# A three-stage attention and feed-forward kernel: a first product row in plain fp32, one division moved from GpSimd to VectorE, and three orders changed

## The chip, the cores and the metric

The kernel runs on one core of one Trainium2 chip. The time is the device time of one launch in microseconds (us). The kernel before takes 1252.05 us, the median of three runs (1251.96, 1252.05, 1252.21).

## The reference

Two inputs, x (8 batches, 8 heads, 512 tokens, 64 wide) and 32 states per batch and head, attend to each other in both directions. The 4352 rows of the result (512 + 32 per batch) go through two feed-forward layers. All is fp32.

```python
def _attn_ref(x, state):
    scores = scale * np.matmul(x, state.transpose(0, 1, 3, 2))      # tokens read states
    a = np.exp(scores - scores.max(-1, keepdims=True))
    a /= a.sum(-1, keepdims=True) + 1e-09
    xread = np.matmul(a, state)
    scores2 = scale * np.matmul(state, x.transpose(0, 1, 3, 2))     # states read tokens
    a2 = ...                                                        # the same softmax
    sread = np.matmul(a2, x)
    return np.concatenate([xread, sread], axis=2)

def _moe_ref(x, w1, w2, w3, w_out):       # 512 -> 1024 -> 1024 -> 512
    return (((x @ w1) * (x @ w2)) @ w3) @ w_out

def _moe2_ref(x, w_in, w_out):            # 512 -> 2048 -> 512
    h = x @ w_in
    return (h - np.tanh(h)) @ w_out
```

## The kernel before, in words

Most matrix products are done in three passes of fp32r: each operand is split into a high part (ScalarE copies it to fp32r) and a low part (VectorE subtracts the high part from the whole), and TensorE adds hi·hi, hi·lo and lo·hi. A product that is not split is written in plain fp32.

The program has four stages.

- **The front** (`stage_front`). It folds w3 @ w_out into one matrix `w34` (1024 x 512) in eight rows of 128, and between the rows it does the attention of the states, one batch e after the other. On TensorE batch e is `scores(e)` (L658, plain fp32), three pieces of product row e (`piece`, L699, 6 matmuls each), `sread_turn(e-1)` (L686), `a2_turn(e)` (transposes, L666), the last piece, `sread(e)` (L678). Row 0 and batch 0 stand ahead of this loop in an order of their own, with transposes of an identity in between (`warm`, L641, and `fill`, L646) that compute nothing that is used.
- ScalarE in batch e: `copy_st` (L474, scores out of PSUM), `exp_a2` (L482), `split_sr(e-1)` (L501), `turn_a2` (L490), `split_w3(e+1)` (L451, high part), `empty_prod(e)` (L462), `copy_sr` (L497). From e = 6 also `split_w` (L470).
- VectorE in batch e: `tokens_max` (L573 and L575, the row maximum that the exponential needs), `tokens_invert` (L581, L583), `split_sr(e-1)` (L588), `split_w3(e+1)` (L552, low part), `empty_prod(e)` (L562). In batches 2 to 5 the softmax of the other direction for batch 0 (the class `Rows`) stands in this list: `vector_turn` and `vector_max` at e = 2, `vector_sub` at 3, `vector_sum` (L167) and `vector_invert` (L172, L174) at 4, `vector_back` (L183) at 5. The product with 1/sum between the last two (L179) is GpSimd's.
- `stage_ys` and `stage_moe1` do the states' product and then, for each batch b, the first feed-forward network with w34. Here too `Rows` prepares the batch after the next, its last step at f = 7 of the eight steps f of a batch.
- `stage_moe2` does the second network and stores the result. The last act is the states' rows: eight stores of 64 KB, four from SyncE's queue (half 0) and four from ScalarE's (half 1, after VectorE's last copy, L1327).

What sets the order: each engine runs its own list in the order in which it is written, and waits on semaphores. No scheduler moves anything. Loads are issued by SyncE in the order of `sync`, each after the wait that frees its place: `load_xT(e)` (L375) waits for `scores`, `load_xs(e)` (L381) for `sread`, `load_w3(r)` (L391) for product row r-2 in its buffer of two.

Of the kernel before, what the change touches and what calls it, by code (L numbers as in the profile page):

```python
# [32 lines left out]
P = 128  # L33
# [39 lines left out]
WARM = 36  # L73
# [59 lines left out]
class Rows:  # L133
# [161 lines left out]
def stage_front(nc, sem, room_a, room_b, room_c, room_o, small, w_at, x_rows, x_cols, state_cols, w1, w2, w3_cols, wo, aT, w34_at, w34,  # L295
# [56 lines left out]
    sT_in, xT_in, xs_in = ([sem(f"{x}_in{n}") for n in range(2)] for x in ("sT", "xT", "xs"))  # L352
    w_hi, w_lo = sem("w_hi"), sem("w_lo")
    w3_in, w3_hi, w3_lo = [sem(f"w3_in{n}") for n in range(2)], sem("w3_hi"), sem("w3_lo")
    first_in = [sem(f"first_in{n}") for n in range(2)]
# [77 lines left out]
    def gpsimd(pool):  # L433
# [5 lines left out]
        for e in range(B):  # L439
            rows.gpsimd_scale(pool, e)  # L440

    def scalar(act):
        def split_first(n):
            act.wait_ge(first_in[n], 16)
            act.activation(w3T[0][0][:, FIRST[n], :], w3r[0][:, FIRST[n], :], ACT.Copy).then_inc(w3_hi, 1)

        def split_w3(r):
            act.wait_ge(w3_in[r % 2], 16 * ((r + 1) // 2))

            after(act, prod_done, r - 1)  # L450
# [6 lines left out]
        def empty_prod(r):  # L457
            act.wait_ge(prod_done, r + 1)
# [85 lines left out]
    def vector(dve):  # L544
        def split_first(n):
            dve.wait_ge(w3_hi, n + 1)
            dve.tensor_tensor(w3T[1][0][:, FIRST[n], :], w3r[0][:, FIRST[n], :], plain(w3T[0][0][:, FIRST[n], :]), ALU.subtract
                              ).then_inc(w3_lo, 1)

        def split_w3(r):  # L550
            dve.wait_ge(w3_hi, r + 2)
# [3 lines left out]
        def split_wo(n):  # L555
            dve.wait_ge(wo_hi, n + 1)
# [863 lines left out]
```

## Time and profile before

| | value |
|---|---|
| median of three runs | 1252.05 us |
| time of the profiled execution | 1251.81 us |
| its span, first to last instruction | 1249.6 us |
| TensorE matmul busy | 1239.4 us, 99% of the span |
| TensorE weight load busy | 1007.1 us, 81% |
| VectorE busy | 795.6 us, 64% |
| ScalarE busy | 548.3 us, 44% |
| GpSimd busy | 16.0 us, 1%, 14 instructions |
| DMA, first tenth of the span | 374, 403, 117 and 21 GB/s in four slices of 31 us |

The span is what the profiler saw between the first and the last instruction of the execution; the time has 2.2 us more around it. TensorE is busy in all of the 40 slices of the page. Its busy share says little of its own rate, since matmuls overlap in the record; what matters in the rows below is when each group of its instructions starts.

### The profile page before, as it was taken

How to read it: one execution, taken by the hardware profiler on the slowest of the kernel's cores; microseconds unless marked ns; L12 is line 12 of the kernel's file. 1: busy time of each engine (PE TensorE's matmuls, PEld its weight loads, DVE VectorE, ACT ScalarE, POOL GpSimd, SP SyncE). 2: the span in 40 equal slices, each digit the busy share in tenths (PEclk: the TensorE clock that was granted, in tenths of full speed). 3: DMA queues.
4: the chain of work that ended last, by engine and by line, in shares of the span. 5: the costliest groups of instructions: out<-in, count | busy, mean ns of one | idle time of the engine just before them, and what ended most of it. 6: DMA issues, size and time to landing. Idle time of an engine off the chain costs nothing. (4 is left out here: it accounts for less than half of the span.)

```text
span 1249.6 us, 17133 instructions
## 1 busy us (share of the span) xinstructions
PE 1239.4 (99%) x6652; PEld 1007.1 (81%) x6652; DVE 795.6 (64%) x1282; ACT 548.3 (44%) x1023; POOL 16.0 (1%) x14
## 2 busy tenths in 40 slices
PE   9999999999999999999999999999999999999998
PEld 6779777777777778888888888888888888888887
DVE  4656556555555444878676676676676776776766
ACT  5663333333333334555444444444444444443443
POOL 0000000000000000000000000000000000000000
PEclk9999999999999999999999999999999999999999
DMA  9930100000000111221101001001001001010000
GB/s 374 403 117 21 65 34 1 35 34 1 34 35 1 68 53 66 93 58 35 51 17 37 16 18 51 1 18 50 0 17 50 8 9 50 17 42 0 8 35 17
DMA packets 18109, 63.75 MB, mean 51 GB/s; under 512 B 1920, under 2 KB 3200, under 8 KB 14080
## 3 DMA queue, kind: packets, MB, share of 16 engines
q1 hardware_dynamic: 17712, 62.59, 13.7%
q8 instruction: 40, 0.66, 0.2%
q10 hardware_dynamic: 336, 0.33, 0.1%
q14 instruction: 21, 0.17, 0.0%
HBM read 45.09 MB, written 17.83 MB: 50 GB/s over the span
## 5 line engine op out<-in xcount | busy, mean ns | idle before, releaser
L1213 ACT ACTIVATE hq<-bank 128x512 f32<-128x512 f32 (+1 forms) x144 | 82.8, 575 | 395.8 <-PE bank L1339 395.8
L1284 DVE TENSOR_TENSOR hw<-hw,hq 128x512 f32<-128x512 f32 (+1 forms) x144 | 95.5, 663 | 194.9 <-ACT hw L1224 194.7
L1339 PE MATMUL bank<-ysp_hi,wi_lo 128*128 128x512 f32 (+1 forms) x576 | 217.2, 377 | 0.0
L1339 PE MATMUL bank<-ysp_lo,wi_hi 128*128 128x512 f32 (+1 forms) x576 | 217.2, 377 | 0.0
L1339 PE MATMUL bank<-ysp_hi,wi_hi 128*128 128x512 f32 (+1 forms) x576 | 217.2, 377 | 0.0
L1365 PE MATMUL wide<-wz_hi,gsp_hi 128*128 128x512 f32 x544 | 212.5, 391 | 1.4 <-DVE gsp_lo L1274 1.3
L1365 PE MATMUL wide<-wz_hi,gsp_lo 128*128 128x512 f32 x544 | 211.8, 389 | 0.0
L1365 PE MATMUL wide<-wz_lo,gsp_hi 128*128 128x512 f32 x544 | 211.8, 389 | 0.0
L1339 PEld LDWEIGHTS bank<-ysp_lo,wi_hi 128*128 128x128 f32 x576 | 108.3, 188 | 20.7
L1339 PEld LDWEIGHTS bank<-ysp_hi,wi_hi 128*128 128x128 f32 x576 | 108.2, 188 | 20.5
L1339 PEld LDWEIGHTS bank<-ysp_hi,wi_lo 128*128 128x128 f32 x576 | 108.3, 188 | 19.9
L1365 PEld LDWEIGHTS wide<-wz_hi,gsp_hi 128*128 128x128 f32 x544 | 102.2, 188 | 23.5 <-DVE gsp_lo L1274 2.8
L1365 PEld LDWEIGHTS wide<-wz_hi,gsp_lo 128*128 128x128 f32 x544 | 102.1, 188 | 21.4
L1365 PEld LDWEIGHTS wide<-wz_lo,gsp_hi 128*128 128x128 f32 x544 | 102.2, 188 | 20.5
L1274 DVE TENSOR_TENSOR gsp_lo<-gb,gsp_hi 128x512 fp32r<-128x512 f32 (+1 forms) x144 | 95.5, 663 | 13.4 <-ACT gsp_hi L1206 0.5
L1038 PE MATMUL wide<-psp_hi,w_hi 128*128 128x512 f32 x256 | 101.4, 396 | 0.1
L1301 DVE COPY_PREDICATED gb<-far,wide 128x512 f32<-128x512 uint8 (+1 forms) x144 | 100.8, 700 | 0.2
L1038 PE MATMUL wide<-psp_lo,w_hi 128*128 128x512 f32 x256 | 99.8, 390 | 0.0
L1038 PE MATMUL wide<-psp_hi,w_lo 128*128 128x512 f32 x256 | 99.6, 389 | 0.0
L1303 DVE TENSOR_TENSOR gb<-bank,gb 128x512 f32<-128x512 f32 (+1 forms) x144 | 95.3, 662 | 5.0
L1291 DVE SCALAR_TENSOR_TENSOR gb<-hw,bank 128x512 f32<-128x512 f32 (+1 forms) x144 | 93.7, 651 | 0.1
L1206 ACT ACTIVATE gsp_hi<-gb 128x512 fp32r<-128x512 f32 (+1 forms) x144 | 86.1, 598 | 3.3 <-DVE gb L1303 3.2
(127 smaller groups left out, 1754.7 us busy)
## 6 DMA issues: line engine op xcount, KB each, us to landing
y_dram<-ysb SPq DMA_DIRECT2D x8, 1024.0 KB, 3.9
out<-ysb SPq DMA_DIRECT2D x8, 1024.0 KB, 4.6
yr<-y_dram SPq DMA_DIRECT2D x28, 256.0 KB, 4.1
xs<-in_x_rows SPq DMA_DIRECT2D x6, 1024.0 KB, 8.6
xT<-in_x_cols SPq DMA_DIRECT2D x5, 1024.0 KB, 9.9
w_raw<-in_moe_w SPq DMA_DIRECT2D x8, 512.0 KB, 8.2
wi_raw<-in_moe_w_in SPq DMA_DIRECT2D x4, 1024.0 KB, 6.7
raw<-in_moe_w_out SPq DMA_DIRECT2D x16, 256.0 KB, 2.6
```

Source lines behind the costliest of these rows:

```text
L1038: mm = pe.matmul(py[c], w34[s][:, f, c * P:(c + 1) * P], psp[t][:, f % 2, :], start=f + m == 0, stop=f == NF1 - 1 and m == LAST)
L1206: act.activation(gsp[0][:, slot, 0:w], gb[:, slot % 2, 0:w], ACT.Copy).then_inc(g_hi, 1)
L1213: act.activation(hq[:, f % 2, 0:w], ph[f % 2][:, 0:w], ACT.Square).then_inc(sq_done, 1)
L1274: dve.tensor_tensor(gsp[1][:, slot, 0:w], g, plain(gsp[0][:, slot, 0:w]), ALU.subtract).then_inc(g_lo, 1)
L1284: dve.tensor_tensor(u, u, q, ALU.mult).then_inc(w2_done, 1)
L1291: dve.scalar_tensor_tensor(g, u, 1.0, h, ALU.add, ALU.mult).then_inc(near_done, 1)
L1301: dve.copy_predicated(g, far[:, f % 2, 0:w], pq[f % 2][:, 0:w]).then_inc(sel_done, 1)
L1303: dve.tensor_tensor(g, h, g, ALU.subtract).then_inc(g_done, 1)
L1339: mm = pe.matmul(ph[f % 2][:, 0:w], wi[s][c][:, f * P:(f + 1) * P], ysp[k][u][c][:, 0:w], start=c + m == 0, stop=c == KC - 1 and m == LAST)
L1365: mm = pe.matmul(po[j], gsp[s][:, f % 4, j * P:(j + 1) * P], wz[u][:, f, :], start=f + m == 0, stop=f == NF2 - 1 and m == LAST)
```

## The change

Six edits, all of them in the lists of instructions:

1. Row 0 of the product (`first`, new) is made of whole tiles in plain fp32 (8 matmuls of 128x512) in place of 24 in fp32r from split tiles. The splits of w3's row 0 are gone (`split_first`, two instructions each on ScalarE and VectorE). `warm` has 20 transposes, not 36; `fill` 6 after `scores(0)`, not 12 and 4. w_out is still split, since rows 1 to 7 use its parts, but its low part, which is written over the whole one, now waits for `first`.
2. SyncE loads x of batch 0 (`load_xT(0)`) ahead of the second part of w3's row 0, `load_xs(0)` ahead of w3's row 1, and the states in two parts: batch 1 alone ahead of `load_xT(1)`, the rest behind it.
3. `load_w3(2)` goes ahead of `load_xT(2)`, and `load_w3(5)` ahead of `load_xT(6)`.
4. On VectorE `split_w3(e+1)` and `split_sr(e-1)` go ahead of the `Rows` steps of batches 4 and 5.
5. The product with 1/sum (L179) is done by VectorE in all eight batches, directly ahead of `vector_back`.
6. Of the last four stores on ScalarE's queue one is issued by SyncE.

On TensorE, the start of the program, first before and then after the change:

```order
1 L641 MATMUL wide<-ident 128x128 x36
2 L699 MATMUL bank<-wos_hi,w3T_hi_75 128x512
3 L699 MATMUL bank<-wos_lo,w3T_hi_75 128x512
4 L699 MATMUL bank<-wos_hi,w3T_lo_77 128x512
5 L699 MATMUL bank<-wos_hi,w3T_hi_75 128x512
6 L699 MATMUL bank<-wos_lo,w3T_hi_75 128x512
7 L699 MATMUL bank<-wos_hi,w3T_lo_77 128x512
8 L658 MATMUL wide<-xT,sT 32x512 x8
9 L646 MATMUL wide<-ident 128x128 x12
```

```order
1 L641 MATMUL wide<-ident 128x128 x20
2 L693 MATMUL bank<-wor,w3r_79 128x512 x2
3 L658 MATMUL wide<-xT,sT 32x512 x8
4 L646 MATMUL wide<-ident 128x128 x6
5 L693 MATMUL bank<-wor,w3r_79 128x512 x4
6 L666 MATMUL wide<-ident,a_72 128x128 x8
7 L693 MATMUL bank<-wor,w3r_79 128x512 x2
8 L678 MATMUL wide<-xs,a2T 32x64 x32
9 L658 MATMUL wide<-aT,sT 32x512 x8
```

The eight fp32 matmuls from `w3r` and `wor` are all of row 0; the first piece of it comes before `scores(0)` as before, the last before `sread(0)`.

On SyncE, the loads from the start of the program to the third x (before, then after):

```order
1 L400 DMA w3r_79<-in_w_cols 128x256
2 L397 DMA wor<-in_moe_w_out 128x2x512
3 L400 DMA w3r_79<-in_w_cols 128x768
4 L375 DMA xT<-in_x_cols 128x2048
5 L397 DMA wor<-in_moe_w_out 128x2x512 x3
6 L391 DMA w3r_80<-in_w_cols 128x1024
7 L381 DMA xs<-in_x_rows 128x2048
8 L411 DMA sT<-in_state_cols 128x896
9 L375 DMA aT<-in_x_cols 128x2x1024
10 L381 DMA aT<-in_x_rows 128x2x1024
11 L375 DMA xT<-in_x_cols 128x2048 [waits scored]
12 L391 DMA w3r_79<-in_w_cols 128x1024 [waits prod_done]
```

```order
1 L403 DMA w3r_79<-in_w_cols 128x256
2 L400 DMA wor<-in_moe_w_out 128x2x512
3 L375 DMA xT<-in_x_cols 128x2048
4 L403 DMA w3r_79<-in_w_cols 128x768
5 L400 DMA wor<-in_moe_w_out 128x2x512 x3
6 L381 DMA xs<-in_x_rows 128x2048
7 L394 DMA w3r_80<-in_w_cols 128x1024
8 L414 DMA sT<-in_state_cols 128x128
9 L375 DMA aT<-in_x_cols 128x2x1024
10 L416 DMA sT<-in_state_cols 128x768
11 L381 DMA aT<-in_x_rows 128x2x1024
12 L394 DMA w3r_79<-in_w_cols 128x1024 [waits first_done]
```

Row 9 of both is x of batch 1 (into a part of `aT`). The states of batches 2 to 7 (128x768) now stand behind it.

On VectorE, batches 4 and 5 of the front, from the end of `tokens_invert(4)` to `tokens_max(6)` (before, then after):

```order
40 L167 TENSOR_REDUCE rsum<-a_94 128x32
41 L172 TENSOR_SCALAR rsum<-rsum 128x32
42 L174 RECIPROCAL rinv<-rsum 128x32
43 L588 TENSOR_TENSOR srs_lo<-wide,srs_hi 128x4x32
44 L552 TENSOR_TENSOR w3T_lo_78<-w3r_80,w3T_hi_76 128x1024
45 L562 TENSOR_TENSOR w_lo<-bank,w_hi 128x512
46 L573 TENSOR_REDUCE tmax<-aT 128x2
...
50 L183 STREAM_TRANSPOSE aT<-a_94 128x2x512
51 L588 TENSOR_TENSOR srs_lo<-wide,srs_hi 128x4x32
52 L552 TENSOR_TENSOR w3T_lo_77<-w3r_79,w3T_hi_75 128x1024
53 L562 TENSOR_TENSOR w_lo<-bank,w_hi 128x512
54 L573 TENSOR_REDUCE tmax<-aT 128x2
```

```order
39 L589 TENSOR_TENSOR srs_lo<-wide,srs_hi 128x4x32
40 L551 TENSOR_TENSOR w3T_lo_78<-w3r_80,w3T_hi_76 128x1024
41 L167 TENSOR_REDUCE rsum<-a_94 128x32
42 L172 TENSOR_SCALAR rsum<-rsum 128x32
43 L174 RECIPROCAL rinv<-rsum 128x32
44 L563 TENSOR_TENSOR w_lo<-bank,w_hi 128x512
45 L574 TENSOR_REDUCE tmax<-aT 128x2
...
50 L551 TENSOR_TENSOR w3T_lo_77<-w3r_79,w3T_hi_75 128x1024
51 L179 TENSOR_TENSOR a_94<-a_94,rinv 128x1024
52 L183 STREAM_TRANSPOSE aT<-a_94 128x2x512
53 L563 TENSOR_TENSOR w_lo<-bank,w_hi 128x512
54 L574 TENSOR_REDUCE tmax<-aT 128x2
```

The steps of `Rows` (a_94, rsum, rinv) stood ahead of w3's low part and stand now between it and the next `tmax`; L179 is new on this engine.

The diff, cut to its core:

```diff
-WARM = 36
+WARM = 20
-    def gpsimd_scale(self, pool, e):
+    def vector_scale(self, dve, e):
...
     def load_w3(eng, r):
-        after(eng, prod_done, r - 1)
+        if r == 2:
+            eng.wait_ge(first_done, 4)
+        else:
+            after(eng, prod_done, r - 2)
...
-        split_first(0)
         split_wo(0)
-        split_first(1)
+        copy_st(0)
         split_wo(1)
-        copy_st(0)
+        exp_a2(0)
         split_wo(2)
+        turn_a2(0)
         split_wo(3)
-        exp_a2(0)
-        turn_a2(0)
         split_w3(1)
...
         def split_wo(n):
             dve.wait_ge(wo_hi, n + 1)
+            dve.wait_ge(first_done, n + 1)
...
-        split_first(0)
         split_wo(0)
-        split_first(1)
+        tokens_max(0)
         split_wo(1)
-        tokens_max(0)
+        tokens_invert(0)
         split_wo(2)
-        split_wo(3)
-        tokens_invert(0)
         split_w3(1)
         empty_prod(0)
+        split_wo(3)
...
+            split_sr(e - 1)
+            if e < NF1 - 1:
+                split_w3(e + 1)
             if e == 4:
                 rows.vector_sum(dve, 0)
                 rows.vector_invert(dve, 0)
             if e == 5:
+                rows.vector_scale(dve, 0)
                 rows.vector_back(dve, 0)
-            split_sr(e - 1)
-            if e < NF1 - 1:
-                split_w3(e + 1)
             empty_prod(e)
...
+        def first(n):
+            pe.wait_ge(first_in[min(n, 1)], 16)
+            pe.wait_ge(wo_in[n], 16)
+            for k in (2 * n, 2 * n + 1):
+                mm = pe.matmul(pz[0], w3r[0][:, k, :], wor[:, k, :], start=k == 0, stop=k == NF1 - 1)
+            mm.then_inc(first_done, 1)
...
                     if f == 7:
+                        rows.vector_scale(dve, b + 2)
                         rows.vector_back(dve, b + 2)
...
         sp.wait_ge(o_copied, J * B + 1)
         store_states(sp, 0)
+        sp.wait_ge(second_copied, 1)
+        store_states(sp, 1, range(3, P // NS))
...
             act.wait_ge(second_copied, 1)
-            store_states(act, 1)
+            store_states(act, 1, range(3))
```

## Rows read from the trace of the kernel before

**Rows 1.** Busy time by stretch: front, first network (engines, PEclk, DMA share, GB/s)

```profile
20.00:30.00 10.00, 9.63 (x129) 6.70 (x129) 4.09 (x8) 6.30 (x14) 0.00 (x0) 1.00 1.02 414
140.00:160.00 20.00, 20.00 (x112) 15.24 (x111) 11.57 (x15) 8.00 (x12) 0.00 (x0) 1.00 0.00 1
```

**Rows 2.** Timeline, TensorE's weight loads, the start (start, us, instructions, idle before)

```profile
1.53 6.25 PEld L641 LDWEIGHTS wide<-ident 128*128 128x128 f32 x36 [1.53 <-POOL ident L436]
...
10.35 1.30 PEld L646 LDWEIGHTS wide<-ident 128*128 128x128 f32 x12 [0.84 <-issue]
...
20.34 0.21 PEld L658 LDWEIGHTS wide<-aT,sT 64*32 64x32 f32 x16 [0.52 <-issue]
```

**Rows 3.** Timeline, SyncE's queue: when x of batches 0 and 1 is issued

```profile
2.18 0.43 SPq L375 DMA_DIRECT2D xT<-in_x_cols  x1
...
5.99 0.67 SPq L375 DMA_DIRECT2D aT<-in_x_cols  x1
```

**Rows 4.** DMA issues of the first 10 us: size, us to landing

```profile
xT<-in_x_cols SPq DMA_DIRECT2D x1, 1024.0 KB, 6.6
...
aT<-in_x_cols SPq DMA_DIRECT2D x1, 1024.0 KB, 14.3
```

**Rows 5.** Timeline, VectorE, batches 4 to 6 of the front

```profile
52.86 1.22 DVE L167 TENSOR_REDUCE rsum<-a 128x32 f32<-128x1024 f32 x1 [0.58 <-ACT a L163]
...
54.60 0.23 DVE L588 TENSOR_TENSOR srs_lo<-wide,srs_hi 128x128 fp32r<-128x128 f32 x1
54.94 2.82 DVE L552 TENSOR_TENSOR w3T_lo<-w3r,w3T_hi 128x1024 fp32r<-128x1024 f32 x1
...
58.29 1.20 DVE L573 TENSOR_REDUCE tmax<-aT 128x2 f32<-128x1024 f32 x1
...
61.20 0.17 DVE L581 TENSOR_SCALAR tinv<-tsum 128x2 f32<-128x2 f32 x1 [1.51 <-ACT a L482]
...
61.49 1.22 DVE L183 STREAM_TRANSPOSE aT<-a 128x1024 f32<-128x1024 f32 x1
...
64.90 1.23 DVE L552 TENSOR_TENSOR w3T_lo<-w3r,w3T_hi 128x1024 fp32r<-128x1024 f32 x1 [1.96 <-ACT w3T_hi L451]
66.04 0.68 DVE L562 TENSOR_TENSOR w_lo<-bank,w_hi 128x512 fp32r<-128x512 f32 x1
67.78 1.22 DVE L573 TENSOR_REDUCE tmax<-aT 128x2 f32<-128x1024 f32 x1 [1.06 <-ACT aT L474]
```

**Rows 6.** Timeline, GpSimd, the same stretch

```profile
54.76 1.92 POOL L179 TENSOR_TENSOR a<-a,rinv 128x1024 f32<-128x1024 f32 x1 [53.29 <-DVE rinv L174]
```

**Rows 7.** Timeline, TensorE's weight loads, batches 5 and 6

```profile
55.45 0.18 PEld L658 LDWEIGHTS wide<-xT,sT 64*32 64x32 f32 x16
57.81 0.19 PEld L699 LDWEIGHTS bank<-wos_hi,w3T_hi 128*128 128x128 f32 x1 [2.18 <-DVE w3T_lo L552]
...
62.04 0.91 PEld L666 LDWEIGHTS wide<-ident,a 128*128 128x128 f32 x8
...
65.53 0.18 PEld L658 LDWEIGHTS wide<-aT,sT 64*32 64x32 f32 x16
66.55 0.19 PEld L699 LDWEIGHTS bank<-wos_hi,w3T_hi 128*128 128x128 f32 x1 [0.84 <-DVE w3T_lo L552]
...
70.77 0.90 PEld L666 LDWEIGHTS wide<-ident,a 128*128 128x128 f32 x8
```

**Rows 8.** Timeline, first network, end of batch 0: VectorE

```profile
169.91 0.69 DVE L947 TENSOR_TENSOR pm<-am,bank 128x512 f32<-128x512 f32 x1 [0.22 <-ACT am L881]
171.29 0.69 DVE L949 TENSOR_TENSOR psp_lo<-pm,psp_hi 128x512 fp32r<-128x512 f32 x1 [0.70 <-ACT psp_hi L885]
```

**Rows 9.** Timeline, TensorE: where it takes that psp

```profile
174.52 0.39 PE L1038 MATMUL wide<-psp_hi,w_hi 128*128 128x512 f32 x1
```

**Rows 10.** Timeline, the queues of SyncE and ScalarE at the end

```profile
1245.40 1.75 SPq L1123 DMA_DIRECT2D out<-ysb  x4
1246.13 1.83 ACTq L1123 DMA_DIRECT2D out<-ysb  x4
```

More of the change, by code:

```diff
@@ L351, in stage_front @@
     ident_zeroed, ident_ready = sem("ident_zeroed"), sem("ident_ready")
-    sT_in, xT_in, xs_in = ([sem(f"{x}_in{n}") for n in range(2)] for x in ("sT", "xT", "xs"))
+    sT_in, xT_in, xs_in = ([sem(f"{x}_in{n}") for n in range(3)] for x in ("sT", "xT", "xs"))
     w_hi, w_lo = sem("w_hi"), sem("w_lo")
     w3_in, w3_hi, w3_lo = [sem(f"w3_in{n}") for n in range(2)], sem("w3_hi"), sem("w3_lo")
-    first_in = [sem(f"first_in{n}") for n in range(2)]
+    first_in, first_done = [sem(f"first_in{n}") for n in range(2)], sem("first_done")
     XT_IN = ((0, 1), (1, 1), (0, 2), (1, 2), (0, 3), (0, 4), (1, 3), (0, 5))
@@ L403, in sync @@
         load_wo(0)
+        load_xT(sp, 0)
         load_first(1)
-        load_xT(sp, 0)
         load_wo(1)
@@ L408, in sync @@
         load_wo(3)
+        load_xs(sp, 0)
         load_w3(sp, 1)
-        load_xs(sp, 0)
-        sp.dma_start(sT[:, 1:B, :, :], state_cols[:, 1:B, :, :]).then_inc(sT_in[1], 16)
+        sp.dma_start(sT[:, 1:2, :, :], state_cols[:, 1:2, :, :]).then_inc(sT_in[1], 16)
         load_xT(sp, 1)
+        sp.dma_start(sT[:, 2:B, :, :], state_cols[:, 2:B, :, :]).then_inc(sT_in[2], 16)
         load_xs(sp, 1)
         for e in range(2, 5):
+            if e == 2:
+                load_w3(sp, e)
             load_xT(sp, e)
-            load_w3(sp, e)
+            if e > 2:
+                load_w3(sp, e)
             for n in ((0,), (1, 2), (3,))[e - 2]:
@@ L419, in sync @@
             load_xs(sp, e)
+        load_w3(sp, 5)
         load_xT(sp, 6)
-        load_w3(sp, 5)
         load_xT(sp, 5)
@@ L437, in gpsimd @@
                            base=0, pattern=[[-1, P]], channel_multiplier=1).then_inc(ident_ready, 1)
-        for e in range(B):
-            rows.gpsimd_scale(pool, e)
     def scalar(act):
-        def split_first(n):
-            act.wait_ge(first_in[n], 16)
-            act.activation(w3T[0][0][:, FIRST[n], :], w3r[0][:, FIRST[n], :], ACT.Copy).then_inc(w3_hi, 1)
         def split_w3(r):
             act.wait_ge(w3_in[r % 2], 16 * ((r + 1) // 2))
-            after(act, prod_done, r - 1)
+            if r == 2:
+                act.wait_ge(first_done, 4)
+            else:
+                after(act, prod_done, r - 2)
             act.activation(w3T[0][r % 2][:, :, :], w3r[r % 2][:, :, :], ACT.Copy).then_inc(w3_hi, 1)
@@ L457, in empty_prod @@
         def empty_prod(r):
-            act.wait_ge(prod_done, r + 1)
+            if r == 0:
+                act.wait_ge(first_done, 4)
+            else:
+                act.wait_ge(prod_done, r)
             if r == 6:
@@ L648, in scores @@
         def scores(e):
-            if e < 2:
+            if e < 3:
                 pe.wait_ge(sT_in[e], 16)
@@ L726, in tensor @@
         warm()
-        piece(0, 0)
+        first(0)
         scores(0)
-        fill(12)
-        piece(0, 1)
-        fill(4)
-        piece(0, 2)
+        fill(6)
+        first(1)
+        first(2)
         a2_turn(0)
-        piece(0, 3)
+        first(3)
         sread(0)
@@ L782, in vector @@
         rows.vector_invert(dve, 1)
+        rows.vector_scale(dve, 1)
         rows.vector_back(dve, 1)
@@ L1119, in width, with store_states @@
         return NSTATE if states(t) else W
-    def store_states(eng, j):
-        for n in range(P // NS):
+    def store_states(eng, j, batches=range(P // NS)):
+        for n in batches:
             eng.dma_start(out_v[j * (P // NS) + n, S:ROWS, :], ob[n * NS:(n + 1) * NS, j, :]).then_inc(o_out, 16)
```

16 lines of the change are left out of this document (5 added, 11 removed).

## The prediction

> **What bounds the kernel now.** I read the table of busy time first, then the stretches, then the lists of single engines where TensorE is not full. TensorE is the bound. In the first network it has no free moment (20.00 us busy of 20.00); in the front it is short of full by a few tenths (9.63 of 10), and there the DMA engines are full as well: 1.02 of their time, 414 GB/s [rows 1]. So an edit can pay in three places only: where TensorE waits in the front, where the first loads land, and behind the last matmul. The reader should see four things.
>
> - The start. 36 identity transposes take 6.25 us; one at full speed is 1.30 / 12 = 0.109 us [rows 2]. At twice that while the clock is at 1.2 GHz, n slow ones solve 0.218 n + 0.109 (36 - n) = 6.25, n = 21: the clock rises some 4.7 us after the first, near 6.2.
> - The first wait that counts. x of batch 1 is issued at 5.99 and lands 14.3 later, at 20.29 [rows 3, 4]; `scores(1)` starts at 20.34 [rows 2]. That start is set by the loads, not by the work before it.
> - Batch 5. `scores(5)` starts at 55.45 and the next product piece at 57.81, 2.36 later; in batch 6 the same step takes 1.02 (65.53 to 66.55) [rows 7]. TensorE waits 1.34 us for w3's low part. That instruction took 2.82 us against 1.23 for its twin in the next batch [rows 5], and it overlaps GpSimd's product, 54.76 to 56.68 [rows 6].
> - The end. The fourth store of half 1 is the last thing issued, about 1.4 us into ScalarE's 1.83 of issuing [rows 10].
>
> On the third point a rule bears. The Trainium skill, page "SBUF — State Buffer", section "Who interferes with whom", says that a VectorE instruction with two inputs in SBUF and a GpSimd instruction that reads SBUF exclude each other for the whole of an instruction. By that rule the low part would end at 56.68 + 1.23 = 57.9; the trace has 57.76, so it agrees, and the stall goes when the product leaves GpSimd.
>
> **The change part by part.** The sum is made against the profiled execution (span 1249.6, time 1251.81, 2.2 around the span); the median of the runs is 0.24 above that time.
>
> *Row 0 in fp32 and the loads of the start.* What ends last is x of batch 1, so count bytes ahead of and with it in SyncE's queue. Before: 128 + 512 + 384 + 1024 + 1536 + 512 + 1024 + 448 + 1024 = 6592 KB, landed 20.29. x of batch 0 (2048 KB in all) landed at 2.18 + 6.6 = 8.78 [rows 3, 4]. That is 4544 KB in 11.5 us, 395 KB per us. After: the states of batches 2 to 7 (384 KB) stand behind it, 6208 KB: 0.97 us sooner, 19.3.
>
> Is TensorE there by then? 20 transposes at 0.218 end at 5.9. An fp32 matmul of 128x512 is not in the trace alone. From above: `scores` is eight such matmuls on eight separate parts of the array at once, 1.02 us [rows 7]. From below: a transposed identity of 128 columns is one pass of fp32 in 0.109, so one pass over 512 columns is 0.44 and no product needs less than one. I take two passes, 0.87, near the upper row, as the record counts 16 weight loads for those eight matmuls [rows 7]. Two matmuls end at 5.9 + 1.74 + 0.3 for the last of the slow clock = 7.9; `scores(0)` has its x at 8.78 - 0.97 = 7.8 and ends at 8.9; the fills 9.6; w_out's second quarter lands at 8.8 + 512 / 395 = 10.1; four matmuls end at 13.6, eight transposes 14.5, two matmuls 16.3, `sread(0)` 17.4. At 1.02 each `sread(0)` would end at 18.6 (8 x 0.15 more), at 0.44 sooner. All are ahead of 19.3, so neither the dearer row 0 nor the missing fills cost anything: the cover is the wait for x. The splits taken off ScalarE and VectorE lie under the same wait. Term: -0.97, bounds -1.5 and 0.
>
> *The order of w3's second and fifth rows.* TensorE moves 0.97 sooner, yet the bytes ahead of later loads are the same and the queue is full, so those land when they did. `load_xT(2)` stands now behind a wait for row 0, which ends at 16.3, while the queue holds 7616 KB by then, work until 8.8 + 5568 / 395 = 22.9: no gap. Each batch takes 1024 KB of x twice, 512 of w3 and 512 to 1024 of w1 and w2, 3072 to 3584 KB or 7.8 to 9.1 us at 395 KB per us, against 8.7 of TensorE (62.04 to 70.77 is 8.73 [rows 7]). The lead can so shrink, by up to all of it. I take 0 lost and keep +0.97 as a bound.
>
> *VectorE, batches 4 and 5.* Times here are those of before, unshifted. Removed: the stall of 1.34. Added: what stands between w3's low part and the next `tmax`. `tmax` is due 2.25 after `scores` starts (67.78 - 65.53 [rows 5, 7]) and VectorE is idle 1.06 before it. The exponentials are done 2.91 after `tmax` starts (58.29 to 61.20), and `a2_turn` stands 5.24 after `scores` (65.53 to 70.77), against 2.25 + 2.91 = 5.16 at best. The spare is 0.1: a late `tmax` is paid by TensorE almost in full.
>
> Batch 4: low part at 54.94 as before but 1.14 to its successor (64.90 to 66.04), then sum, guard and reciprocal 54.60 - 52.86 = 1.74, then `empty_prod` 0.68 less an overlap of 0.09: `tmax(5)` at 54.94 + 1.14 + 1.74 + 0.59 = 58.41, due at 55.45 + 2.25 = 57.70. Late by 0.71, so `a2_turn(5)` is at 58.41 + 2.91 + 0.05 = 61.37, against 62.04 before. So far -0.67.
>
> Batch 5: the low part follows `a2_turn` by 64.90 - 62.04 = 2.86. Then 1.14, the product (1.23 and 0.03 of semaphore, as the next instruction needs its result), the transpose back (1.22 - 0.08), `empty_prod` 0.60: `tmax(6)` at 61.37 + 2.86 + 1.14 + 1.26 + 1.14 + 0.60 = 68.37. `scores(6)` starts 3.49 after `a2_turn(5)`, 64.86, so `tmax(6)` is due at 67.11: late by 1.26. `a2_turn(6)` comes at 68.37 + 2.91 + 0.05 = 71.33, against 70.77 before. Term: +0.56. What moved away from TensorE's w3 wait comes back as a wait for the exponentials. Bounds: -1.34 (lateness costs nothing) and +0.9.
>
> *The product on VectorE in the first network.* Per batch 1.26 at the last step. With the split of w_in behind it (batches 0 and 1) the next `pm` starts some 0.4 late: before, it sat idle 0.22, and psp is 0.6 sooner without GpSimd. The low part of that psp would start at 171.7 and end at 172.4 [rows 8]; TensorE takes it at 174.52 [rows 9]. Hidden by 2.1 us in each batch. Term 0, bounds 0 and 10 (eight times 1.26).
>
> *The end.* SyncE has issued its four stores at 1245.40 + 1.75 = 1247.15 and can issue the eighth at once, where ScalarE did it at 1246.13 + 3 x 0.46 = 1247.5 [rows 10]. Term: -0.3, bounds -0.46 and 0.
>
> Sum: -0.97 + 0.56 + 0 - 0.3 = -0.7. The span comes to 1248.9, the profiled time to 1251.1, the median to 1251.4.
>
> **The rivals.**
>
> *A. The late tmax costs nothing.* If the exponentials had more room than I read, the sum is -0.97 - 1.34 - 0.3 = -2.6, a median of 1249.4. For it: in batch 5 of before `tmax` was late too (58.29 against 57.70) and no separate wait shows. Against: there TensorE was itself 1.34 late.
>
> *B. The loads take the lead back.* Somewhere in batches 2 to 5 a load lands as before and TensorE waits for it. Then only 0.56 - 0.3 is left: a median of 1252.3. For it: the DMA share of 1.02 [rows 1]. Against: 7.8 us of loads in most batches stand against 8.7 of TensorE, so the loads gain on it.
>
> *C. The clock.* TensorE would stand idle from 17.4 to 19.3. In the start above, about 4.7 us of work went at half speed before the clock rose. If it falls in this gap, 4.7 us at half speed lose 2.35: a median of 1253.8, slower. It decides at whether the granted clock in the stretch from 17 to 25 us is under 1. In the rows the clock is 1.00 from 20 to 30 us [rows 1], right behind an idle 0.52 [rows 2]. The Trainium skill, "TensorE: Matmul & The Clock Gate", section "What's actually happening", says that the throttled state is the default and activity lifts it, so idling speaks against the change; no row of before has a gap this long.
>
> *D. VectorE becomes the bound in the first network.* If the 2.1 us of cover were missing, up to 8 x 1.26: a median near 1262. Only if `pm` of step 0 is more than 2.1 late.
>
> **How the numbers follow.** Forecast 0.58, A 0.14, B 0.19, C 0.06, D 0.03. The predicted time is 1251.4. About 2.5 us (0.2%) is what a measurement of this kernel can tell from no change, so faster needs 1249.5 or less: half of A, and a little of the forecast's edge (a lead of 1.5 with lateness half paid), 0.10. Slower needs 1254.6 or more: D and the upper part of C, 0.05. Same is 0.85. The range goes from just under A's 1249.4 to between B and C: 1249.2 to 1252.9.
>
> **What would show it.** `scores(1)` at 19.3, behind a gap of nearly 2 us, with x of batch 1 landing at that moment. w3's low parts of rows 5 and 6 in 1.23 each and no wait of TensorE for them. In their place a wait before `a2_turn` (the transposes of `a`) of 0.6 in batch 5 and 1.2 in batch 6, released by the exponentials, with `tmax` running late by 0.7 and 1.3. PEclk 1.00 from 6.3 on. The first network full, as before. The last store on SyncE near 1246.5. It is wrong if `scores(1)` to `scores(7)` takes less than before (A), if waits for loads appear in batches 2 to 5 (B), or if a row of the start shows a clock under 1 (C).

## The result, and the profile after

The changed kernel takes 1253.5 us, the median of 20 runs (1252.82 to 1257.99); the kernel before, on the same chip, 1252.07 (20 runs, 1251.75 to 1253.22). The ratio is 1.0013, with a 95% interval of 1.0007 to 1.0019: 1.4 us slower, where 0.7 us faster was forecast. The profiled execution took 1254.15 with a span of 1252.4, against 1251.81 and 1249.6. So what is compared below is 2.7 us of span (2.8 from the rounded values). What lies outside the span, first instruction to last, shrank: 2.15 us before on average, 1.80 in the changed kernel. So by the medians the time is 1.4 longer and the span 1.8.

Stretches of the changed kernel (columns as in [rows 1]: engines, PEclk, DMA share, GB/s):

```profile
17.00:21.00 4.00, 2.09 (x81) 1.15 (x80) 2.54 (x3) 2.11 (x5) 0.00 (x0) 1.00 1.03 407
20.00:30.00 10.00, 9.81 (x85) 7.30 (x89) 3.56 (x8) 4.94 (x10) 0.00 (x0) 0.83 1.02 414
21.30:24.60 3.30, 3.30 (x8) 2.63 (x9) 1.51 (x3) 1.74 (x4) 0.00 (x0) 0.50 1.04 421
24.60:40.00 15.40, 15.40 (x219) 11.45 (x218) 8.07 (x14) 9.84 (x22) 0.00 (x0) 1.00 1.02 411
46.00:48.00 2.00, 2.00 (x70) 1.46 (x68) 0.78 (x2) 1.81 (x3) 0.00 (x0) 1.00 0.33 135
140.00:160.00 20.00, 20.00 (x113) 15.23 (x112) 12.98 (x16) 8.87 (x14) 0.00 (x0) 1.00 0.00 0
```

Rows two and three are the surprise: the granted clock is 0.50 (1.2 GHz) from 21.3 to 24.6 us. [rows 1] had 1.00 over the same ten microseconds. The last row shows the first network full, as before. The fifth has the DMA engines two thirds idle in a stretch where the kernel before had 0.99. The column PEclk says 1.00 for the first microseconds too, where 20 transposes take 4.13 us, 0.21 each against 0.11 later; so it tells nothing of the start.

The fall is not in every execution, and not in the median. At 0.50 for 3.3 us it takes 0.0013 off the mean clock of an execution. 12 of the 20 executions have a mean clock of 1.000, so they had no such fall, and their median is 1253.48. Four have 0.998 or less: 1254.03 and 1254.15, which is the profiled one, and 1257.34 and 1257.99, which lost more than this fall explains.

TensorE's weight loads of the front, changed kernel (start, us, instructions, idle before), which answer to [rows 2] and [rows 7]:

```profile
17.18 0.94 PEld L678 LDWEIGHTS wide<-xs,a2T 128*32 128x32 f32 x64 [0.76 <-issue]
20.16 0.21 PEld L658 LDWEIGHTS wide<-aT,sT 64*32 64x32 f32 x16 [2.04 <-issue]
...
24.36 0.33 PEld L705 LDWEIGHTS bank<-wos_hi,w3T_lo 128*128 128x128 f32 x1
24.74 0.19 PEld L705 LDWEIGHTS bank<-wos_hi,w3T_hi 128*128 128x128 f32 x1
...
27.01 0.90 PEld L666 LDWEIGHTS wide<-ident,a 128*128 128x128 f32 x8
...
56.74 0.18 PEld L658 LDWEIGHTS wide<-xT,sT 64*32 64x32 f32 x16
57.76 0.19 PEld L705 LDWEIGHTS bank<-wos_hi,w3T_hi 128*128 128x128 f32 x1 [0.84 <-DVE w3T_lo L551]
...
62.59 0.86 PEld L666 LDWEIGHTS wide<-ident,a 128*128 128x128 f32 x8 [0.70 <-ACT a L488]
...
67.06 0.19 PEld L705 LDWEIGHTS bank<-wos_hi,w3T_hi 128*128 128x128 f32 x1 [0.84 <-DVE w3T_lo L551]
...
72.48 0.86 PEld L666 LDWEIGHTS wide<-ident,a 128*128 128x128 f32 x8 [1.28 <-ACT a L488]
```

`scores(1)` starts at 20.16 behind an idle of 2.04, not at 19.3. Behind it one weight load takes 0.33 and then, at 24.74, 0.19 again: that is the clock. `a2_turn(1)` is at 27.01, 25.66 before. In batch 5 the step from `scores` to the next piece is 1.02 now (56.74 to 57.76), so the wait for w3's low part is gone. In its place stand the two waits for the exponentials, 0.70 and 1.28 on this list. `a2_turn` comes at 53.25, 62.59, 72.48 and 81.19, where before it came at 51.95, 62.04, 70.77 and 79.52.

VectorE, the same batches, which answers to [rows 5]:

```profile
56.22 1.23 DVE L551 TENSOR_TENSOR w3T_lo<-w3r,w3T_hi 128x1024 fp32r<-128x1024 f32 x1 [1.63 <-ACT w3T_hi L454]
...
59.65 1.21 DVE L574 TENSOR_REDUCE tmax<-aT 128x2 f32<-128x1024 f32 x1
...
65.41 1.23 DVE L551 TENSOR_TENSOR w3T_lo<-w3r,w3T_hi 128x1024 fp32r<-128x1024 f32 x1 [2.28 <-ACT w3T_hi L454]
66.55 1.22 DVE L179 TENSOR_TENSOR a<-a,rinv 128x1024 f32<-128x1024 f32 x1
...
69.55 1.20 DVE L574 TENSOR_REDUCE tmax<-aT 128x2 f32<-128x1024 f32 x1
```

w3's low part takes 1.23 in both; it was 2.82 beside GpSimd's product. `tmax` is 2.91 (59.65 - 56.74) and 3.51 (69.55 - 66.04) behind `scores`, where 2.25 is in time.

The loop of the second network is where I had predicted nothing at all. The branch at its turn, TensorE's sequencer, first the kernel before and then the changed one (duration min/median/max in ns, when):

```profile
L1383 PEldq COMPARE_BRANCH  x2: 220/232/243, 840.1 to 1014.2; - x2
```

```profile
L1392 PEldq COMPARE_BRANCH  x2: 3619/3736/3852, 841.8 to 1016.3; - x2
```

And the DMA queue that brings instructions, whole program, before and after (packets, MB, share):

```profile
q8 instruction: 40, 0.66, 0.2%
```

```profile
q8 instruction: 58, 0.95, 0.3%
```

18 packets more of 16 KB: nine between the two turns (842 to 1010 us, where before has none) and nine from the second turn on. From the first matmul of this network (503.51 before, 505.23 after) to the first of its last step (1237.76, 1240.48) it is 734.25 and 735.25 us.

So the 2.7 us of this profile are: start -0.2, the clock +1.5, batch 5 -0.75 and batch 6 +1.16, the first network 0 (1.67 late at 81.19, 1.72 at its end), the loop +1.0, the end 0. Without the clock 1.2 is left, where the median span is 1.8 longer. The other 0.6 is not in this profile and stays open; the wait of `scores(5)` for x, 0.35 to 1.6 us in four profiles below and 0 in this one, would be of the size, but no run shows it for this kernel.

### The profile page after: what moved, and what is told of

Same layout as the page of the kernel before. It is cut to its first block and busy times, and to the rows that moved or that the text cites. A ratio compares the mean times of both kernels' runs of the same rounds, so it can differ in the third digit from the quotient of the medians.

```text
span 1252.4 us, 17068 instructions
## 1 busy us (share of the span) xinstructions
PE 1240.9 (99%) x6618; PEld 1003.5 (80%) x6618; DVE 798.8 (64%) x1288; ACT 547.2 (44%) x1021; POOL 0.7 (0%) x6
## 5 line engine op out<-in xcount | busy, mean ns | idle before, releaser
L1348 PEld LDWEIGHTS bank<-ysp_lo,wi_hi 128*128 128x128 f32 x576 | 108.3, 188 | 20.5
```

The source lines that it names most:

```text
L1348: mm = pe.matmul(ph[f % 2][:, 0:w], wi[s][c][:, f * P:(f + 1) * P], ysp[k][u][c][:, 0:w], start=c + m == 0, stop=c == KC - 1 and m == LAST)
```

## The experiments

Each was timed in five rounds (11 runs); `a_late` was run once. The kernel before took 1252.15, 1252.09 and 1252.24 beside the three sets. Position means the number of an instruction in TensorE's stream, counted in the compiled program (no trace shows it); the second network's loop starts at 8172 before and at 8106 in the changed kernel, and is 1576 instructions long. Where a wait of TensorE is given without a row it is read from its list of matmuls, which shows less idle time than the list of weight loads in the rows.

**a_pad: the position alone.** The changed kernel with waits that are met already, which move the loop.

```diff
         warm()
+        for _ in range(68):
+            pe.wait_ge(ident_ready, 1)
         first(0)
```

> The changed kernel with 68 more waits on a semaphore that is long set, in 34 instructions, behind the first transposes of TensorE's list. They compute nothing and lie under 4.4 us of transposes; they move the loop of the second network 34 places back in TensorE's instruction stream, from 8106 to 8140 (before it stood at 8172). Theory R (where the loop stands in the stream decides whether it has to be fetched again at each turn): the two turns' branches take 0.2 us as before, not 3.6 and 3.9, the loop's start-up gaps go, and the time is 1.0 us under the changed kernel's 1253.5, 1252.5. Rival N (the two long branches came from elsewhere, or the waits cost time of their own): the branches stay at 3.6 to 3.9, and the time at 1253.5 or above. Both expect the gap of 1.9 before scores(1), and the clock at 0.5 for 3.4 us behind it in some executions, a wait of 0.6 in batch 5 and of 1.15 in batch 6.

1252.92 (1251.61 to 1254.53), ratio 1.0005 (0.9996 to 1.0014). The loop starts at 8140.

```profile
L1394 PEldq COMPARE_BRANCH  x2: 220/229/238, 842.6 to 1016.7; - x2
```

The branch is short again and the network takes 734.19. This execution had the clock at 0.50 from 21.3 to 24.6 too, and a loss of its own:

```profile
58.15 0.18 PEld L658 LDWEIGHTS wide<-xT,sT 64*32 64x32 f32 x16 [1.76 <-DMA xT<-in_x_cols]
```

`scores(5)` waits for x of batch 5, which was rival B. That, and the fall of the clock (four of these 11 executions have a mean clock of 0.998, three have 1.000), may be why the gain is 0.6 in the median and not 1.0. The three without a fall took 1252.04, 1252.27 and 1252.38, 1.2 below the changed kernel's 1253.48.

**a_fill: the gap filled.** Work of no use in the gap before `scores(1)`; it moves the loop to 8140 as well, so it is to be held against a_pad.

```diff
         sread(0)
+        fill(17)
```

> The changed kernel with 17 more transposes of the identity between sread(0) and scores(1), 1.85 us of work that fills the gap of 1.9. They are 34 instructions too, so the loop stands at 8140 as with the waits. Theory C (the clock fell because TensorE stood idle there): the granted clock is 1.00 from 20 to 30 us in the profile and 1.000 in all executions, scores(1) starts at 20.2 still, a2_turn(1) at 25.4 and not at 27.0; the time is 1.5 under the kernel with the waits where that one's clock fell, 0.5 to 1.5 in the median, some 1251.5, and the spread of the executions is down to some 0.3. Rival (the clock falls for another reason, such as the lighter load of plain fp32 matmuls before it): the clock falls still, and the two kernels with 34 more instructions are within 0.3 of each other.

1251.77 (1251.39 to 1252.42), ratio 0.9996 (0.9987 to 1.0005), 1.15 below a_pad, and its runs lie within 1.0 us where a_pad's spread over 2.9. No mean clock is under 0.999. Not all of the 1.15 is the clock: a_pad's three executions without a fall have a median of 1252.27, 0.5 above a_fill, and in the two profiles the wait for x is 1.6 and 0.86. What makes that part isn't shown.

```profile
18.30 1.84 PEld L646 LDWEIGHTS wide<-ident 128*128 128x128 f32 x17
20.30 0.18 PEld L658 LDWEIGHTS wide<-aT,sT 64*32 64x32 f32 x16 [0.17 <-issue]
...
56.19 0.18 PEld L658 LDWEIGHTS wide<-xT,sT 64*32 64x32 f32 x16 [1.02 <-DMA xT<-in_x_cols]
```

```profile
21.30:24.60 3.30, 3.30 (x22) 2.74 (x15) 1.57 (x3) 1.61 (x2) 0.00 (x0) 1.00 1.03 416
```

`scores(1)` starts no sooner and the clock stays at full. The three kernels with the gap of 2 us (the changed one, a_pad, a_rows) have a PEclk of 0.83 from 20 to 30 us in their profiles; the eleven with the gap filled or shorter (1.52 us at most on the same list, in b_div_store) have 1.00. The fall does not come at a fixed distance from the gap: in the changed kernel and in a_pad `scores(1)` starts at 20.16 and 19.87 and the clock falls near 21.3, in a_rows it starts at 20.06 and the clock falls at 20.3:

```profile
20.30:23.60 3.30, 3.30 (x20) 1.42 (x5) 1.55 (x2) 1.02 (x1) 0.00 (x0) 0.50 1.04 417
```

**b_div: the product alone.** The kernel before with the product by 1/sum on VectorE ahead of the transpose back, all orders as before.

```diff
-        for e in range(B):
-            rows.gpsimd_scale(pool, e)
...
             if e == 5:
+                rows.vector_scale(dve, 0)
                 rows.vector_back(dve, 0)
...
                     if f == 7:
+                        rows.vector_scale(dve, b + 2)
                         rows.vector_back(dve, b + 2)
```

> The kernel before with one of the six edits: the product with 1/sum done by VectorE, in the old order (in batch 5 right ahead of the transpose back, w3's low part behind it). TensorE's list is untouched. Theory P (GpSimd's product held VectorE's low part of row 5 up, and the product on VectorE has room in the 1.96 us that it is idle before the low part of row 6): no wait of 1.3 in batch 5, none in batch 6; 1.35 faster, 1250.7, ratio 0.9989. Rival (VectorE has no room for eight more instructions of 1.23): a2_turn or the next product piece is late somewhere, and the time is 1252.1 or more.

1250.64 (1250.2 to 1250.83), ratio 0.9988 (0.9978 to 0.9997). VectorE in batch 4:

```profile
54.91 1.23 DVE L550 TENSOR_TENSOR w3T_lo<-w3r,w3T_hi 128x1024 fp32r<-128x1024 f32 x1
56.05 0.68 DVE L560 TENSOR_TENSOR w_lo<-bank,w_hi 128x512 fp32r<-128x512 f32 x1
57.67 1.22 DVE L571 TENSOR_REDUCE tmax<-aT 128x2 f32<-128x1024 f32 x1 [0.94 <-ACT aT L472]
```

No wait of TensorE's matmuls is left between 50 and 82 us, and VectorE is idle 0.94 before `tmax` starts. The whole stall of 1.34 goes with this one edit: the median span is 1.3 shorter (1248.7 for 1250.0). The other 0.2 of the gain lies outside the span, 1.93 us for 2.15 on average; why the time there shrinks isn't shown. Edit 4, the new order in batches 4 and 5, was not needed for it and spends the room that `tmax` had.

**a_rows: the order alone.** a_pad with edit 4 undone.

```diff
-            split_sr(e - 1)
-            if e < NF1 - 1:
-                split_w3(e + 1)
             if e == 4:
...
+            split_sr(e - 1)
+            if e < NF1 - 1:
+                split_w3(e + 1)
             empty_prod(e)
```

> The changed kernel with the 68 waits, and on VectorE the steps of the other softmax in batches 4 and 5 back ahead of the low part of w3, with the product still on VectorE. Theory T (what stands between w3's low part and the next tmax makes the exponentials late): the waits of 0.6 and 1.15 before a2_turn(5) and a2_turn(6) go, from a2_turn(4) to a2_turn(5) and on to a2_turn(6) are 8.73 each, 1.7 us under the kernel with the waits alone, some 1250.8. Rival (the batches are late for loads or for something else): the two distances stay above 9.3 and 9.8, and the time is the same as with the waits alone.

1250.8 (1250.02 to 1254.11), ratio 0.9992 (0.9983 to 1.0001): 2.1 below a_pad, its profiled execution 2.2. The waits for the exponentials, 0.34 and 0.92 in the changed kernel, are gone:

```profile
53.14 0.90 PEld L666 LDWEIGHTS wide<-ident,a 128*128 128x128 f32 x8
57.05 0.18 PEld L658 LDWEIGHTS wide<-xT,sT 64*32 64x32 f32 x16 [0.51 <-DMA xT<-in_x_cols]
62.30 0.91 PEld L666 LDWEIGHTS wide<-ident,a 128*128 128x128 f32 x8
71.03 0.90 PEld L666 LDWEIGHTS wide<-ident,a 128*128 128x128 f32 x8
```

From 62.30 to 71.03 it is 8.73, as expected; from 53.14 to 62.30 it is 9.16, since `scores(5)` still waits for x. In a_pad's profile only the wait of 0.92 is there, as the one for x, 1.6, covers the first; here the one for x is 0.35. It varies from run to run, so what the order alone is worth is known only as 0.9 to 1.3 by the waits.

**a_fill_rows: gap and order together.** a_fill with edit 4 undone, so both of these:

```diff
-            split_sr(e - 1)
-            if e < NF1 - 1:
-                split_w3(e + 1)
             if e == 4:
...
         sread(0)
+        fill(17)
```

> The changed kernel with 17 identity transposes in the gap behind sread(0) (as in a_fill) and with w3's low part of the next row again ahead of the row step in batches 4 and 5, the product on VectorE. The theory that the order of these steps costs the two waits for the exponentials (0.34 and 0.92 us in the changed kernel): they go, and the time is 1.75 us less than a_fill's 1251.77, 1250.0. As the second network's loop starts at the same place in TensorE's stream as in a_fill, its turns take 0.24 us. The rival, that the time so won is taken by the wait of scores(5) for x of batch 5 (0.86 us in a_fill): 1250.9, and a_fill's wait grows from 0.86 towards 1.7.

1250.91 (1249.94 to 1252.42), ratio 0.999 (0.9981 to 0.9999): 0.86 below a_fill, the time of the rival. The wait for the exponentials (0.92 in a_fill's profile, where the one for x covers the first) is gone and the one for x grew from 0.86 to 1.1, so it took back 0.2 and not the 0.9 of the rival; the 1.75 of the theory counted a wait that was not there:

```profile
PE wide L658 <- DMA xT<-in_x_cols: 1.1, 1, 1.1
```

**a_fill_rows_order: the pair of loads.** The same with `load_xT(6)` again ahead of `load_w3(5)`.

```diff
+        load_xT(sp, 6)
         load_w3(sp, 5)
-        load_xT(sp, 6)
         load_xT(sp, 5)
```

> a_fill_rows with one pair of loads back in the old order: x of batch 6 ahead of w3's row 5. The theory that this pair makes scores(5) wait: SyncE's queue holds x of batch 6 while w3's row waits for its buffer, so the DMA share from 46 to 48 us is near 1 (0.33 in the changed kernel), x of batch 5 lands before it is wanted, and the time is 0.3 to 0.9 us less than a_fill_rows: 1249.4. The rival, that the bytes ahead of x of batch 5 are the same and its landing with them: the wait stays and the time is a_fill_rows' within 0.2.

1249.99 (1249.53 to 1250.32), ratio 0.9982 (0.9973 to 0.9991): 0.92 less. SyncE's queue in a_fill_rows, and then here:

```profile
37.83 0.33 SPq L381 DMA_DIRECT2D xs<-in_x_rows  x1
45.52 0.33 SPq L394 DMA_DIRECT2D w3r<-in_w_cols  x1
45.89 0.55 SPq L375 DMA_DIRECT2D aT<-in_x_cols  x1
```

```profile
38.10 0.33 SPq L381 DMA_DIRECT2D xs<-in_x_rows  x1
39.16 0.55 SPq L375 DMA_DIRECT2D aT<-in_x_cols  x1
45.94 0.34 SPq L394 DMA_DIRECT2D w3r<-in_w_cols  x1
```

In the new order w3's row waits for its buffer until 45.5 and x of batch 6, which could go at 39.2, waits behind it. The queue runs low, and 1 MB more then stands in the way of x of batch 5. With the old order the DMA share from 46 to 48 us is 0.98 and the wait is gone.

**b_shift and b_shift_less: the position, in the kernel before.** Waits that are met already, ahead of each product of layer 1 in the first network: 6 of them in b_shift (192 instructions, loop at 8364, which is 8106 + 258), 4 in b_shift_less (128, loop at 8300).

```diff
             n = NF1 * b + f
+            for _ in range(6):
+                pe.wait_ge(values.v_lo, 1)
             if f == 0:
```

> The kernel before with 6 waits that are met already ahead of each product of the first network's layer 1: 192 more instructions in TensorE's stream, no work. The second network's loop starts at instruction 8364 of TensorE's stream in place of 8172, which against blocks of 256 instructions is where the changed kernel has it (8106, 8364 = 8106 + 258). The theory that the place of the loop in the instruction stream costs the 1.05 us in the changed kernel's second network: the branch at the loop's turn takes about 3.6 us in place of 0.24, TensorE stands 0.05 to 0.3 us behind it at most turns, and the time is 1.0 above before: 1253.1. The rival, that the loss came from something that the change does (a load, a semaphore): 1252.1, and branches of 0.24.

> The same as b_shift with 4 waits ahead of each product: 128 more instructions, the loop at 8300. By the theory of the place this is a good one: branches of 0.24, 1252.1. The rival, that the added waits themselves, or a longer stream, cost: two thirds of what b_shift loses, 1252.8.

b_shift 1253.91 (1253.22 to 1255.06), ratio 1.0013 (1.0004 to 1.0022); b_shift_less 1252.06 (1251.7 to 1252.22), ratio 0.9999. The branch in the one and in the other:

```profile
L1385 PEldq COMPARE_BRANCH  x2: 3360/3387/3414, 840.7 to 1015.5; - x2
```

```profile
L1385 PEldq COMPARE_BRANCH  x2: 220/232/243, 840.3 to 1014.3; - x2
```

```profile
q8 instruction: 59, 0.97, 0.3%
```

```profile
q8 instruction: 41, 0.67, 0.2%
```

64 instructions that do nothing, ahead of the loop, make 1.17 us in it (735.40 against 734.23), and nothing of the change is in these kernels. b_shift lost 1.85 in all. 0.5 of that lies in the front of its profiled execution, whose code is that of before: against b_shift_less `scores(1)` starts 0.2 later (20.62 for 20.44), and the wait for w3's low part at 30.8 is 0.3 longer; I have no cause for it.

**b_store and b_div_store: the end.** One of ScalarE's four last stores on SyncE, alone, and on top of b_div.

```diff
         store_states(sp, 0)
+        sp.wait_ge(second_copied, 1)
+        store_states(sp, 1, range(3, P // NS))
...
-            store_states(act, 1)
+            store_states(act, 1, range(3))
```

> The kernel before with one of ScalarE's four last stores on SyncE and nothing else. By the prediction -0.3: 1251.8. By the rival of b_div_store: 1252.1.

> b_div (the kernel before with the product of the row division on VectorE) with one of ScalarE's four last stores on SyncE. The prediction had -0.3 for the store: 1250.3 against b_div's 1250.64, with the last store issued 0.46 sooner. The rival, that the end is set by something else than the issue of the fourth store: 1250.6. The changed kernel's own trace speaks for the rival: its last matmul and its end are late by the same amount.

1252.09 (1251.78 to 1253.0) against 1252.24, and 1250.54 (1250.17 to 1251.35) against b_div's 1250.64. The queues at the end of b_store, which answer to [rows 10]:

```profile
1245.51 2.24 SPq L1123 DMA_DIRECT2D out<-ysb  x5
1246.25 1.36 ACTq L1123 DMA_DIRECT2D out<-ysb  x3
```

The issuing ends at 1247.75 where before it ended at 1247.96, and the whole list is 0.1 later here: 0.3 sooner. Yet the span ends 4.8 us (before) and 4.9 us (here) behind the start of ScalarE's last copy (L1198 before, L1200 here). So the shorter list of issues is not what ends last. The medians are 0.15 and 0.1 lower, within what they can tell.

**a_late: what stands behind x of batch 1.** a_fill_rows_order, with SyncE issuing nothing behind this load until it has landed.

```diff
         load_xT(sp, 1)
+        sp.wait_ge(xT_in[1], 16)
```

> a_fill_rows_order with one wait more: SyncE issues nothing behind x of batch 1 until that has landed. It measures what the transfers behind it cost it. In a_fill_rows_order x of batch 1 landed at about 20.3, when some 0.3 to 0.4 MB behind it had already moved. The theory that these bytes take its share of the DMA engines: it lands 0.5 to 0.9 sooner, near 19.5, and scores(1) waits only for the identity transposes (they end at 20.4). The rival, that the landing goes by the bytes ahead alone: 20.3 as in a_fill_rows_order. The queue runs dry behind it, so the whole is slower in both, by 1 to 2 us.

One run, 1252.12. Issues of the first microseconds (size, us to landing), a_late:

```profile
aT<-in_x_cols SPq DMA_DIRECT2D x1, 1024.0 KB, 13.3
```

It was issued at 6.68 and landed at 19.98; in the changed kernel at 6.75 and 20.05, also 13.3 later. a_fill_rows_order's 20.35 had its issue at 7.05, so the 0.4 less is all in the issue. The rival holds: bytes behind a load cost it no more than the 0.1 that these rows resolve, in one profile.

**a_first: the first loads.** a_fill_rows_order with the second part of w3's row 0 again ahead of x of batch 0, 8 transposes in the gap and 28 waits that keep the loop at 8136.

```diff
         load_wo(0)
+        load_first(1)
         load_xT(sp, 0)
-        load_first(1)
```

> a_fill_rows_order with w3's row 0, second part, again ahead of x of batch 0 in SyncE's queue, 8 identity transposes in the gap in place of 17, and 28 waits that are met already, so that the second network's loop stands where it did (8140). In the first 12 us the queue moved 3.73 MB before and 3.61 MB in the changed kernel. The theory that the new order of the first loads costs this (0.12 to 0.15 MB, 0.3 to 0.4 us at 0.4 MB per us): 3.7 MB or more in the first 12 us, x of batch 1 lands near 19.7, and as later batches stand at the loads too, the time is 0.3 below a_fill_rows_order's 1249.99: 1249.7. The rival, that the smaller amount comes from elsewhere: 3.6 MB, and 1250.0. x of batch 0 lands 0.4 to 0.7 later, which costs nothing while sread(0) still ends before x of batch 1 lands.

1249.46 (1249.3 to 1249.87), ratio 0.9978 (0.9969 to 0.9987). It is the fastest of all, 2.8 under the kernel before, and 0.53 below a_fill_rows_order (timed beside another set). x of batch 0 landed at 9.08, x of batch 1 at 19.68:

```profile
18.14 0.85 PEld L646 LDWEIGHTS wide<-ident 128*128 128x128 f32 x8
19.71 0.21 PEld L658 LDWEIGHTS wide<-aT,sT 64*32 64x32 f32 x16 [0.71 <-issue]
```

The amounts moved in the first 12 us, for before, the changed kernel and a_first:

```profile
DMA packets 1642, 3.73 MB, mean 310 GB/s; under 512 B 117, under 2 KB 373, under 8 KB 1514
```

```profile
DMA packets 1581, 3.61 MB, mean 301 GB/s; under 512 B 114, under 2 KB 370, under 8 KB 1451
```

```profile
DMA packets 1600, 3.64 MB, mean 303 GB/s; under 512 B 112, under 2 KB 368, under 8 KB 1472
```

The landing came as expected and the amount did not: 3.64, not 3.7. a_pad, with the changed kernel's order, even moved 3.70. How much of the landing is the order's is not shown: with the changed kernel's order x of batch 1 landed at 19.78 to 20.35 in seven profiles, and 19.68 is one profile. The run has a second edit that bears on the time, 8 transposes for 17. They end at 19.0 here; 17 of them would hold `scores(1)` until 20.15 (in a_late they start at 18.15 and `scores(1)` at 20.16), however early x landed. By that estimate up to 0.44 of the 0.53 needs the shorter fill. No run separates the two.

## Why the prediction was wrong, step by step

The median came out 2.1 us above the forecast. In the median the steps that failed are two: the sum had no term for the place of the loop (1.0), and its terms for the start and the end, -0.97 and -0.3, came to -0.24 and 0. The clock comes on top in the executions where it falls, the profiled one among them.

- **The place of the loop (no term, no rival).** 1.0 us in the profile, and 1.2 between the executions without a fall of the changed kernel and of a_pad. The sum had each edit's work and none for what the edits do to the length of TensorE's stream: 66 instructions fewer ahead of the loop. a_pad takes it away without touching any work, b_shift brings it into the kernel before, b_shift_less does not. That the place decides is shown; why it does is not. The Trainium skill, "Runtime: NRT & Kernel Launch", section "Instruction fetch mechanics", says that instructions come in blocks of 16 KB (256 of them), that TensorE's buffer holds 2048, and that a taken branch stalls on a fetch when its target is outside a window of two blocks. The packets of 16 KB in the trace agree. The window of two does not: by it this loop would stall at each turn wherever it stands, and in the kernel before the branch takes 0.23 us with no packet between the turns. An estimate from that page's figures: the loop of 1576 instructions lies in seven blocks or, at some positions, in eight, and eight are the whole buffer. Which positions those are I did not test beyond the two bad ones (8106, 8364) and the four good ones (8136, 8140, 8172, 8300).
- **The clock (rival C, chance 0.06).** The prediction put it in numbers: 2.35 us if the clock falls in the gap from 17.4 to 19.3. It fell, and cost 1.5 in the profiled execution: `a2_turn(1)` is 1.35 late though `scores(1)` is 0.18 early. It was a rival with a chance, so not a term that was left out, and the median without a fall is 1253.48 all the same. I held the fall unlikely, since the clock was 1.00 behind an idle 0.52 [rows 2], a gap a quarter as long. That the gap does it is shown by a_pad against a_fill; it falls in part of the executions, 4 to 8 of the 20 by their mean clocks (0.999 can be either). The Trainium skill, "TensorE: Matmul & The Clock Gate", section "HAM oscillation — how this bites in real kernels", gives as its abstract rule a longer idle than this one as what to avoid; here an idle of 2.0 us went before the fall, so the measurement decides: a shorter gap can cost it too. The gap itself was foreseen (nearly 2 us); its price was not.
- **Row 0 and the loads of the start (term -0.97).** It was -0.24. The fp32 matmul was right: two weight loads 0.43 apart, 0.86 for each matmul at full clock (forecast 0.87), and `sread(0)` ended before x of batch 1, as the prediction had it. The landing was wrong, and in its first half only. From x of batch 0 to x of batch 1 it took 11.58 us (8.47 to 20.05) for the same 4544 KB that took 11.51 before. But 384 KB less ahead of x of batch 0 brought that 0.31 sooner (8.47 for 8.78), not 0.97. This is the term that was mis-sized: bytes taken out there were not worth 1/395 us per KB. In the first 4 us the queue is not at its full rate (119 GB/s before and 103 in the changed kernel, against 418 and 397 in the next 4), and by 8 us the changed kernel had moved 0.15 MB less (250 for 269 GB/s), some 0.4 us of the missing 0.66. The rest stays open. Both landings vary by execution: over all 14 profiles x of batch 0 lands at 8.8 to 9.1 with the old order of the first loads (a_first included) and at 8.3 to 8.9 with the new one, x of batch 1 at 20.3 to 20.5 (once 21.5, in b_div_store) with the loads of before and at 19.8 to 20.35 with the new ones. So the term is 0.2 to 0.4.
- **The order of w3's rows (0 forecast, bound +0.97).** 0 in the changed kernel's own profile and 0.35 to 1.6 in four others; 0.92 in the medians (a_fill_rows against a_fill_rows_order). I looked at row 2 and the start for gaps in the queue, and not at row 5, where SyncE waits from 39.7 to 47.06. This is rival B in part: a load takes the lead back, but through an idle queue, not a full one.
- **VectorE in batches 4 and 5 (term +0.56).** The mechanism and both sizes were right: late by 0.66 and 1.26 (forecast 0.71 and 1.26), and batch 5 at 9.34 for 10.09 (-0.75; forecast -0.67), batch 6 at 9.89 for 8.73 (+1.16; forecast +1.23). `tmax` was late and TensorE paid for it, so rival A falls.
- **GpSimd's lock.** Right: 1.23 for 2.82, in the changed kernel and in b_div alone.
- **The product in the first network (0).** Right. psp's low part is done at 174.03 and TensorE takes it at 176.23, 2.2 of cover (forecast 2.1). Rival D falls.
- **The end (-0.3).** Mis-sized: from the last step of the second network to the end of the span it is 11.9 us in both, and at most 0.15 in the medians of b_store and b_div_store. What ends last is not the issue of the eighth store; what it is stays open.

Forecast 1251.4; with the loop's 1.0, the start's 0.73 and the end's 0.3 that did not come, and 0.41 in place of 0.56 on VectorE, it would have been 1253.3 where the clock does not fall, against 1253.5. That this comes so near is luck in part: it leaves out the 0.35 us that the time outside the span shrank by and some 0.6 inside it that the profile of the changed kernel does not have.

## What to carry to other kernels

Price an idle gap of the matmul engine by what the clock may do behind it, not only by its length, and fill it with work of no use when it can't be closed: 17 identity transposes took the fall away here, 1.15 us in the median with what else came along. But size the fill to what the gap surely is: when x landed early, at 19.98 in a_late, they held `scores(1)` until 20.16. When a kernel has a loop in TensorE's stream, look at the branch at its turn and at the instruction queue's packets after every edit, since an edit elsewhere can move the loop. And an edit that removes a stall often needs only one of its parts: b_div, one engine for one product, gave 1.5 us, and the five edits around it lost that and 1.4 more. With the gap filled, the loop moved, edit 4 undone and two pairs of loads put back (a_first) what is left of them is worth 1.2 below b_div.

## What the runs showed of the hardware that I had not expected

- The same network with the same work takes 734.2 or 735.3 to 735.4 us, by where its loop starts in TensorE's stream: the branch takes 0.23 or 3.4 to 3.9 us, with 9 more packets of 16 KB a turn. TensorE hides most of that behind work that is queued; only 0.3 of the 1.0 shows as idle on its list of matmuls.
- The granted clock fell to 0.50 behind an idle of 2.0 us: at 21.3 in the profiles of the changed kernel and of a_pad, 1.1 and 1.4 us after the idle ended, until 24.7; in a_rows at 20.3, 0.2 us after it ended. It fell in part of the executions, and in no profile with an idle of 1.52 or less.
- A load landed no sooner when nothing stood behind it (13.3 us from issue in both, one profile each).
- With the product off GpSimd the time outside the span is 1.87 to 1.97 us in b_div's executions, where before has 2.15 on average.
